# Attention, routed experts and a mixer on one core: shares stored as rows, and work moved around the first gather

## The reference

```python
# 1: attention of 8 heads of 64, plain within |i - j| < 4, plus attention on means of 4 tokens
out_d = sm_attn(q_d, k_d, v_d); out_up = np.repeat(out_d, factor, axis=2)
attn_out = out_up + out_local
# 2: one of 8 experts per token; a token keeps the expert before it where its gate is >= 0.5
e = fresh_e if s == 0 or local_gate[b, s] < 0.5 else prev_e
p = softmax(logits[b, s])
out[b, s] = p[e] * (np.maximum(x[b, s] @ w1[e], 0.0) @ w2[e])
# 3: a mixer over tokens, then over channels
h = np.maximum(xt @ w_tok1, 0.0) @ w_tok2; u = x + h.T
return u + np.maximum(u @ w_ch1, 0.0) @ w_ch2
```

## Time and profile before

| | us |
|---|---|
| median of 3 runs (lowest, highest) | 935.54 (933.09, 939.22) |
| profiled execution | 937.33 |
| its span | 935.6 |
| TensorE busy in the span | 864.2 |
| VectorE, ScalarE, GpSimd busy | 453.7, 349.0, 232.5 |

### The profile page before, as it was taken

One profiled execution on the slowest core, in us unless ns is written; L12 is line 12 of the kernel. 1 busy time (PEld: TensorE's weight loads), 2 busy tenths in 40 slices (PEclk: granted clock), 3 DMA queues, 4 the chain that ended last, 5 costly groups with the idle time before them and its releaser, 6 DMA issues.

```text
span 935.6 us, 13425 instructions
## 1 busy us (share of the span) xinstructions
PE 864.2 (92%) x4498; PEld 720.4 (77%) x4499; DVE 453.7 (48%) x892; ACT 349.0 (37%) x874; POOL 232.5 (25%) x356
## 2 busy tenths in 40 slices
PE   5889889787699979999999978999999999999998
PEld 3666767656478868888887866899989989999997
DVE  6896978878653434255563537412122353122211
ACT  5666776755153433345563433111111121111110
POOL 6886876763322122221221220000000000000000
PEclk9999999999599989999999997999999999999999
DMA  9658785530161945164554614001001020000000
GB/s 158 114 95 198 151 175 113 150 108 11 52 210 63 196 151 186 46 214 159 197 189 138 199 48 147 1 1 67 2 11 58 1 68 1 1 34 1 34 1 34
DMA packets 98703, 88.41 MB, mean 94 GB/s; under 512 B 67808, under 2 KB 73568, under 8 KB 98656
## 3 DMA queue, kind: packets, MB, share of 16 engines
q1 hardware_dynamic: 94816, 75.22, 30.0%
q0 software_dynamic: 3840, 12.59, 4.5%
HBM read 72.31 MB, written 15.48 MB: 94 GB/s over the span
## 4 chain that ended last, share of the span: by engine, by line
PE 71%; DVE 13%; DMA 5%; issue 4%; POOL 3%; ACT 2%; SPq 1%; POOLq 0%; DVEq 0%; ACTq 0%
PE bank L1625 16%; PE bank L1627 16%; PE bank L1626 16%; PE bank L1683 4%; PE bank L1684 4%; PE bank L1690 4%; DVE xT L1129 2%; PE bank L1674 2%; DVE aT L1107 2%; DMA y_dr<-ysb,snow 2%; DVE kB L1072 2%; DVE nm L1085 1%; PE bank L1463 1%; DMA stage<-in_moe_w 1%; PE bank L1633 1%
## 5 line engine op out<-in xcount | busy, mean ns | idle before, releaser
L1356 DVE SCALAR_TENSOR_TENSOR h2l<-bank,h2h 128x384 fp32r<-128x384 f32 x72 | 40.2, 559 | 190.0 <-ACT h2h L1010 190.0
L1010 ACT ACTIVATE h2h<-bank 128x384 fp32r<-128x384 f32 x72 | 35.4, 492 | 229.7 <-PE bank L1627 229.7
L1625 PE MATMUL bank<-uTh,W 128*128 128x384 f32 x288 | 98.1, 340 | 0.0
L1626 PE MATMUL bank<-uTl,W 128*128 128x384 f32 x288 | 97.5, 338 | 0.0
L1627 PE MATMUL bank<-uTh,W 128*128 128x384 f32 x288 | 97.1, 337 | 0.0
L1627 PE MATMUL bank<-W,h2l 128*128 128x512 f32 x216 | 84.5, 391 | 0.0
L1625 PE MATMUL bank<-W,h2h 128*128 128x512 f32 x216 | 84.3, 390 | 0.0
L1626 PE MATMUL bank<-W,h2h 128*128 128x512 f32 x216 | 84.1, 389 | 0.0
L1683 PE MATMUL bank<-W,hTh 128*128 128x512 f32 x184 | 77.4, 420 | 0.0
L1305 DVE TENSOR_TENSOR W<-stage,W 128x1024 fp32r<-128x1024 f32 x56 | 66.6, 1220 | 20.8 <-ACT W L959 20.6
L1311 DVE TENSOR_TENSOR hTl<-bank,hTh 128x512 fp32r<-128x512 f32 x46 | 31.8, 691 | 91.9 <-ACT hTh L968 91.9
(11 more groups left out here) (218 smaller groups left out, 1812.9 us busy)
## 6 DMA issues: line engine op xcount, KB each, us to landing
stage<-in_moe_w SPq DMA_DIRECT2D x56, 512.0 KB, 4.6
vl<-in_v SPq DMA_DIRECT2D x40, 128.0 KB, 3.7
qraw<-in_q SPq DMA_DIRECT2D x32, 144.0 KB, 5.4
kraw<-in_k SPq DMA_DIRECT2D x32, 144.0 KB, 5.0
v<-in_v SPq DMA_DIRECT2D x8, 576.0 KB
ub<-y_dr SPq DMA_DIRECT2D x18, 256.0 KB, 4.7
out<-ob SPq DMA_DIRECT2D x18, 256.0 KB, 2.6
x_dr<-xrow SPq DMA_DIRECT2D x16, 256.0 KB, 3.7
```

What stands on the lines that cost most here:

```text
L1010: act.activation(dst, bank[bk][:, 0:width], ACT.Relu).then_inc(relu_hi, 1)
L1356: dve.scalar_tensor_tensor(dst, bank[bk][:, 0:width], 0.0, hi.bitcast(F32), ALU.max, ALU.subtract).then_inc(bank_free, 1)
L1625: pe.matmul(ps, ah, bh, start=first, stop=False)
L1626: pe.matmul(ps, ah, bl, start=False, stop=False)
```

## The change

1. The last head pair keeps two of its seven halves (in units 1 and 4). ScalarE makes its five later ones (`LATE_SPLITS`) behind the exponentials of the shares, VectorE three behind the first gather's indices and two behind `x_lo(0)`. TensorE starts expert 0 with the first eight halves (w1) and waits for the others before its down products.
2. `best_of(0)` moves from iteration 70 to 73, `choose(0)` and `less_max(0)` behind the loop. In the drain the three pieces of logits stand together, ahead of rows 1 and 2.
3. The code is multiplied in with `hot_lane`, as second operation of the comparison, no longer into `hot_col`. VectorE makes 18 lanes, GpSimd six.
4. `keep_busy(3)` before the marks are turned, `keep_busy(8)` behind the sums.
5. Shares are computed behind the late halves. TensorE turns them before expert 6, ScalarE copies them and stores 24 rows of 96; SyncE reads 18 rows of 128, TensorE turns them, ScalarE copies them to `prob`. Experts 6 and 7 stand behind the loop over pairs. `t2h` is made behind expert 6 on ScalarE. GpSimd's memsets and first extra gather wait for what they need in a new order: the gather for `route_done`, the memsets for `prob_done`.

```diff
@@ side_work
-                work += [("logits", b, 0), ("rows", b, 1), ("logits", b, 1), ("logits", b, 2), ("rows", b, 2)]
+                work += [("logits", b, 0), ("logits", b, 1), ("logits", b, 2), ("rows", b, 1), ("rows", b, 2)]
@@ split_work
-    if hb == NHB - 1 and u < 7:
-        return [9 + u]
+    if hb == NHB - 1 and u in (1, 4):
+        return [9 + (1, 4).index(u)]
...
+LATE_SPLITS = [range(11, 14), range(14, 16)]
...
-DVE_LANES = 17
+DVE_LANES = 18
@@ SyncE
-            sp.wait_ge(prob_done, 1)
-            sp.dma_start(p_dr.rearrange("(k p) -> p k", p=QP), shares[:, :, :].rearrange("p b t -> p (b t)"),
-                         allow_slow_non_contiguous=True).then_inc(p_out, 16)
...
-            sp.dma_start(prob[:, :], p_dr.rearrange("(t p) -> p t", p=P), allow_slow_non_contiguous=True
-                         ).then_inc(p_in, 16)
+            sp.dma_start(probT[:, :], p_dr.rearrange("(t p) -> t p", p=P)).then_inc(p_in, 16)
@@ GpSimd
-                pool.tensor_scalar(hot_lane[:, k, :], lane_row[0:QP, :], lane[:, k:k + 1], None, ALU.is_equal
-                                   ).then_inc(hot_lane_pool, 1)
+                pool.tensor_scalar(hot_lane[:, k, :], lane_row[0:QP, :], lane[:, k:k + 1], id_code[:, k:k + 1],
+                                   ALU.is_equal, ALU.mult).then_inc(hot_lane_pool, 1)
...
-            pool.wait_ge(prob_done, 1)
+            pool.wait_ge(route_done, 1)
             pool.wait_ge(xg_turned, 1)
             gather(1, 0)
+            pool.wait_ge(prob_done, 1)
@@ ScalarE
             act.activation(ex[:, :, :], lm[:, :, :], ACT.Exp).then_inc(ex_done, 1)
+            for cs in LATE_SPLITS:
+                for c in cs:
+                    split_hi(c)
...
+            act.wait_ge(shares_turned, 1)
+            act.activation(sharesT[:, :], bank[7][0:NK, 0:QP], ACT.Copy).then_inc(sharesT_done, 1)
+            act.wait_ge(sharesT_done, 1)
+            act.dma_start(p_dr.rearrange("(k p) -> k p", p=QP), sharesT[:, :]).then_inc(p_out, 16)
+
+            expert(E - 2, (1, E - 1))
             act.activation(t2h[:, :, P // 2:P // 2 + S], raw2[:, :, P // 2:P // 2 + S], ACT.Copy
                            ).then_inc(tok_hi, 1)
-
-            expert(E - 2, (1, E - 1))
...
+            act.wait_ge(prob_turned, 1)
+            act.activation(prob[:, :], bank[7][:, 0:NT], ACT.Copy).then_inc(prob_ready, 1)
@@ VectorE
-                if g == RA + 7:
+                if g == NU + 1:
                     dve.wait_ge(experts_numbered, 1)
                     best_of(0)
-                if g == RA + 8:
-                    choose(0)
-                    less_max(0)
+            choose(0)
+            less_max(0)
...
-            tt(hot_col[:, :, :], hot_col[:, :, :], bc(id_code[:, :].unsqueeze(2), wide), ALU.mult
-               ).then_inc(hot_col_done, 1)
...
             dve.sem_inc(route_done, 1)
+            for c in LATE_SPLITS[0]:
+                split_lo(c)
...
             x_lo(0)
+            for c in LATE_SPLITS[1]:
+                split_lo(c)
+            dve.wait_ge(ex_done, 1)
...
@@ TensorE
                 if g == NU + 5:
+                    pe.wait_ge(route_const, 1)
+                    keep_busy(3, bank[5])
                     turn_marks()
...
             mm.then_inc(summed, 1)
+            keep_busy(8, bank[5])
...
-            pe.wait_ge(raw0_lo, 2 * CPE)
+            pe.wait_ge(raw0_lo, CPE)
...
                     pe.wait_ge(y_copied, j + 1)
+                    pe.wait_ge(raw0_lo, 2 * CPE)
                     down_hi([0, 1])
...
-            with pe.Fori(0, E // 2) as eh:
+            with pe.Fori(0, E // 2 - 1) as eh:
                 expert(2 * eh, 0)
                 expert(2 * eh + 1, 1)
...
+            pe.wait_ge(prob_done, 1)
+            pe.transpose(bank[7][0:NK, 0:QP], shares[:, :, :].rearrange("p b t -> p (b t)"), ident[0:QP, 0:QP]
+                         ).then_inc(shares_turned, 1)
+            expert(E - 2, 0)
+            expert(E - 1, 1)
...
+            pe.wait_ge(p_in, 16)
+            pe.transpose(bank[7][:, 0:NT], probT[:, :], ident[0:NT, 0:NT]).then_inc(prob_turned, 1)
             pe.wait_ge(moe_done, 1)
```

More of the change, by code:

```diff
@@ L139 @@
 KD, KF, KC = DM // P, F // P, CH // P
-SPLIT_AT = {c: w for w, c in enumerate(c for g in range(NU) for c in split_work(g))}
+SPLIT_AT = {c: w for w, c in enumerate([c for g in range(NU) for c in split_work(g)] +
+                                       [c for cs in LATE_SPLITS for c in cs])}
 LAST_TILES = [range(0, 3), range(3, 5), range(5, 6)]
@@ L267, in build @@
         id_high = sb("id_high", M, [QP, KT, B])
-        id_code = sb("id_code", M, [QP, NK], F16)
+        id_code = sb("id_code", M, [QP, NK])
         within = sb("within", M, [QP, E, B])
@@ L273, in build @@
         shares = sb("shares", M, [QP, B, KT])
+        sharesT = sb("sharesT", M, [NK, QP])
+        probT = sb("probT", M, [NT, P])
         gnow = sb("gnow", M, [P, 1], I32)
@@ L407, in build @@
         route_done = sem("route_done")
+        shares_turned, sharesT_done = sem("shares_turned"), sem("sharesT_done")
         p_out, p_in = sem("p_out"), sem("p_in")
+        prob_turned, prob_ready = sem("prob_turned"), sem("prob_ready")
         lm_done, ex_done = sem("lm_done"), sem("ex_done")
@@ L1028, in _ @@
                 hi_mix(m)
+            act.wait_ge(prob_turned, 1)
+            act.activation(prob[:, :], bank[7][:, 0:NT], ACT.Copy).then_inc(prob_ready, 1)
             act.wait_ge(moe_done, 1)
-            act.wait_ge(p_in, 16)
+            act.wait_ge(prob_ready, 1)
             for i in range(NK5):
@@ L1249, in _ @@
             wide = [QP, NK, NSL2]
-            step(tt(hot_col[:, :, :], bc(col_row[0:QP, :].unsqueeze(1), wide), bc(col[:, :].unsqueeze(2), wide),
-                    ALU.is_equal))
-            tt(hot_col[:, :, :], hot_col[:, :, :], bc(id_code[:, :].unsqueeze(2), wide), ALU.mult
-               ).then_inc(hot_col_done, 1)
+            tt(hot_col[:, :, :], bc(col_row[0:QP, :].unsqueeze(1), wide), bc(col[:, :].unsqueeze(2), wide),
+               ALU.is_equal).then_inc(hot_col_done, 1)
             dve.wait_ge(lane_done, 1)
             for k in range(DVE_LANES):
-                dve.tensor_scalar(hot_lane[:, k, :], lane_row[0:QP, :], lane[:, k:k + 1], None, ALU.is_equal
-                                  ).then_inc(hot_lane_dve, 1)
+                dve.tensor_scalar(hot_lane[:, k, :], lane_row[0:QP, :], lane[:, k:k + 1], id_code[:, k:k + 1],
+                                  ALU.is_equal, ALU.mult).then_inc(hot_lane_dve, 1)
             dve.wait_ge(inverted, 1)
@@ L1325, in _ @@
             x_lo(0)
+            for c in LATE_SPLITS[1]:
+                split_lo(c)
+            dve.wait_ge(ex_done, 1)
+            step(dve.tensor_reduce(dn[:, 0, :], ex[:, :, :].rearrange("p t (b e) -> p (t b) e", e=E), AX.X, ALU.add))
+            step(dve.tensor_scalar_add(dn[:, 1, :], dn[:, 0, :], 1e-9))
+            step(dve.reciprocal(dn[:, 2, :], dn[:, 1, :]))
+            step(tt(pex[:, :, :], ex[:, :, :], seq[:, :, :], ALU.mult))
+            step(dve.tensor_reduce(ps_[:, :], pex[:, :, :].rearrange("p t (b e) -> p (t b) e", e=E), AX.X, ALU.add))
+            step(tt(shares[:, :, :].rearrange("p b t -> p t b"), ps_[:, :].rearrange("p (t b) -> p t b", b=B),
+                    dn[:, 2, :].rearrange("p (t b) -> p t b", b=B), ALU.mult))
+            dve.sem_inc(prob_done, 1)
             def expert(e, split):
@@ L1388, in _ @@
             dve.wait_ge(moe_done, 1)
-            dve.wait_ge(p_in, 16)
+            dve.wait_ge(prob_ready, 1)
             for i in range(NK5):
@@ L1560, in weigh, with keep_busy @@
                 mm.then_inc(o_done, 1)
+            def keep_busy(n, bk):
+                for _ in range(n):
+                    pe.matmul(bk[:, :].rearrange("p (r c) -> p r c", r=4), ones_b[:, :],
+                              bc(ident_b[:, :].unsqueeze(1), [P, 4, P]), start=True, stop=True)
             def side_pieces(g):
@@ L1634, in turn_slot @@
                 mm.then_inc(xg_turned, 1)
-            def keep_busy(n):
-                for _ in range(n):
-                    pe.matmul(bank[7][:, :].rearrange("p (r c) -> p r c", r=4), ones_b[:, :],
-                              bc(ident_b[:, :].unsqueeze(1), [P, 4, P]), start=True, stop=True)
-            keep_busy(10)
+            keep_busy(10, bank[7])
             turn_slot(0)
-            keep_busy(6)
+            keep_busy(6, bank[7])
             pe.wait_ge(route_done, 1)
-            pe.wait_ge(raw0_lo, 2 * CPE)
+            pe.wait_ge(raw0_lo, CPE)
             def expert(e, par):
```

11 lines of the change are left out of this document (removed).

## The result

| us | median | lowest to highest | before, same chip | ratio, 95% interval |
|---|---|---|---|---|
| the changed kernel | 927.35 | 925.49 to 929.35 | 934.94 | 0.9906 (0.9879 to 0.9934) |
| once more, another chip | 924.84 | 923.66 to 925.96 | 937.07 | 0.9871 (0.985 to 0.9892) |
| a third time, another chip | 925.13 | 923.47 to 928.76 | 936.55 | 0.9878 (0.9858 to 0.9898) |

The change makes the kernel 0.9 to 1.3% faster: 7.6, 12.2 and 11.4 us in the three comparisons, where 14.2 was forecast. All three medians lie in the forecast's range of 917 to 927.5 us, the first by only 0.15 us; the forecast gain itself was too large in every comparison. Its profiled execution (929.35 us) is the slowest of its five.

The account below looks back on a forecast made before the run. TensorE, busy 864.2 of 935.6 us, was taken as the bound, so only its gaps and low-clock stretches could be won. Terms -4.2 - 1.6 - 0.1 - 0.8 - 7.8 + 0.3 = -14.2 gave 921.3 us, range 917 to 927.5.

Parts of the forecast that it names:

- Attention's end: Last head pair: five of VectorE's seven halves leave and `best_of(0)` moves, -4.2 us to its last copy of weights.
- The clock in the drain: TensorE after attention: without the 2.48 us gap its clock doesn't fall to 1.2 GHz, -1.6 us, bounded by 0.
- Logits before rows and three products: Before the marks are turned: logits 0.5 us earlier, row block and three idle products make TensorE 0.4 late, -0.1 net.
- The codes: Routing: `hot_col` loses its second operation, GpSimd makes six lanes instead of seven, at the mean price, -0.8 us.
- The bound +2.1: Routing's lanes: GpSimd's six all at its slowest price, 1.27 us each, 7.6 us together, costing 2.1 us.
- Late halves and shares: First expert slots: late halves and shares fit into idle time of ScalarE and VectorE, 0 us, far bound +0.7.
- Behind it are its 1.57 us of idle time: VectorE after `x_lo(0)`: 3.5 us more work is covered by idle times of 1.57 and 2.26 us, 3.8 together.
- Shares as rows: Slot at 322.74 us: storing rows instead of single elements removes the scatter's stall, -7.8 us, bounds -8.2 and -5.
- Small additions: Two more transposes on TensorE with waits, +0.3 us; ScalarE's copies and `t2h` lie in time when nothing waits for them.
- The stall stays: Rival: loads of token and expert weights in flight, not the store, held the scatter; +7.8, 929.1 us, chance 0.10.
- The clock falls elsewhere: Rival: TensorE idles before the gather lands, first slot at half speed (2.9 us), 0.9 lost before marks; 925 us, chance 0.12.
- Slower: Rival: the clock falls in the first slot and stays low; at 50 us it costs 25, giving 946 us, chance 0.02.

Follow-up runs that it names:

- e2: The changed kernel with the six operations on shares put back ahead of `x_lo(0)`, behind the first three late halves; 926.14 us, ratio 0.9878.
- e1: The kernel before with only the storage of the shares changed to rows (turned, stored as 24 rows of 96), `t2h` behind expert 6; 932.40 us, ratio 0.9938.
- e7: The changed kernel with the shares stored and read by single elements again, by SyncE ahead of expert 3's loads; 933.04 us, ratio 0.9965.
- e12: The kernel before, run and profiled once more with nothing changed; 937.35 us.

## Why the prediction was right, and where it wasn't

**Attention's end, -4.2: right.** -4.46 in the mean, the same within 0.03 us in all 11 profiles with the edit, between the two bounds.

**The clock in the drain, -1.6: the step failed.** To the first product with `wg` it gave 1.15, since those units run at 2.4 GHz. But "Without the gap I expect no fall" was wrong: the clock fell all the same, 2 to 5 us further on, with TensorE busy, and took the products with `wg` or the idle ones. To the marks 0.30 us went back, net -0.85. A fall was allowed for, here by the bound 0 and in the first slot by a rival of 0.12, but not expected.

**Logits before rows and three products, -0.1: right in the mean only.** The 0.5 from the earlier logits is seen where the clock holds (6.62 to 6.09 us) and lost where it doesn't (6.86, 7.81). The idle products cost up to 0.9 us before the marks, and where they cost nothing they gain 0.4 behind them (7.90 against 8.29 us); over nine and five profiles it is 8.20 against 8.29.

**The codes, -0.8: wrong sign.** The step "I take the mean price, since the loop over 128 elements stays one pass" failed. It is +0.28. GpSimd's median went from 0.70 to 0.90 us an operation, VectorE's lanes from 3.10 / 17 = 0.18 to 4.31 / 18 = 0.24 us. The mean of 0.79 that the prediction took mixes three prices: in the kernel before GpSimd's first two lanes take 1.27 and 0.93 us, beside VectorE's two operations on `hot_col`, the next four 0.70, beside VectorE's lanes, and the last 0.60, alone. So one lane less was worth 0.70 and one `hot_col` operation less some 0.2, against 0.2 us more for each of six. The bound +2.1 was far off: GpSimd's six took 0.97 us in the mean. The rule on blocking of the Trainium skill ("SBUF — State Buffer", who interferes with whom) doesn't set the price beside the lanes: both engines are in them at once, from 244.83 to 249.14, and GpSimd takes 0.87 to 0.91 us there against 0.79 for its last, almost alone. Beside `hot_col`, a VectorE operation with two inputs in SBUF, the trace agrees with it: GpSimd's first takes 1.50 us, 0.71 more than alone, and `hot_col` itself 0.84.

**Late halves and shares, 0: failed, +1.2.** The step was "Behind it are its 1.57 us of idle time". From `xTl` to the first low part it is 2.27 us before and 2.22 in e2, which has two halves between; with the six operations there too it is 5.92. So the idle time covered the halves and nothing of the six. It wasn't free time: it holds the loads of the slot's bounds into registers, with what belongs to them 2.0 us, which aren't counted as busy. They run beside the halves, which wait for nothing, and start only behind the last of the six, each of which waits for the one before (lines at e2). The low parts free the buffers of the ring, the last chunks land later, ScalarE stands before one of them, and with it the `relu` that TensorE waits for 1.08 us: this chain was missing in the prediction, which had the last chunk's wait hidden behind products.

**Shares as rows, -7.8: right for its slot,** which falls from 20.1 to 12.3 us; 5.45 us is what all slots together gained. One step in it was too short, with no cost: the scatter there lands not after the median of 2.8 us but after 6.2 to 6.7; TensorE still doesn't wait for the gather. Given back: 1.2 in the second slot; 1.0 near 470 us, where ScalarE issues the store before its first chunk of expert 7, which the part on small additions had as hidden; 0.8 in the mean of three by the late chunk near 310 us; 0.2 by a slot of 13.05 in one profile, not looked into. Against that 0.8 us came from the slot near 490 us (14.19 and 13.46 before; 13.33, 12.53 and 13.23 changed), not forecast.

**Small additions, +0.3:** from the last slot to the end -0.5, less by 0.8 than forecast; not followed further.

**The rivals.** *The stall stays* is refuted by e1 and e7. Two of its readings were off: of the loads in flight only five of ten landed within 9 us, the others after 10.9 to 15.4, and elsewhere scatters issued beside expert loads land in 3.7 to 4.3 us in five cases, not 2.8. *The clock falls elsewhere* came half true: it fell, not in the first slot (12.6 us in all) but in the drain, with 0.9 lost before the marks as that rival has it, and its 925 us is where two of the three medians lie, by a sum of other terms. *Slower* did not happen.

Together: -14.2 forecast, -10.8 in the profiles. Of the 3.4 us, 1.1 are the codes, 0.8 the clock and the logits up to `lane` (0.9 instead of 1.7), 2.35 the slots and 0.2 the start, less 0.8 at the end and 0.3 in attention. The sum's best end was added wrongly: the terms at their best give 16.1 us and not 18. The range held because what was missed stayed small beside the two terms that came as forecast, the stall and attention's end.

## What to carry to other kernels

An engine's idle time ahead of a loop can hold the loads of the loop's bounds into registers, which no busy share counts. Work that waits for nothing runs beside them; a chain of short operations that wait for each other goes on top in full. Work put ahead of the consumer of a ring of buffers is paid one slot later, on another engine, so follow the buffers and not only the engine. A stall that one long transfer explains could be forecast to the tenth in its own slot, though not in the total; terms around a clock that moves between executions need several profiles of both kernels.

## What the runs showed of the hardware

- TensorE's clock fell to 1.2 GHz with no gap just before it: in the changed kernel TensorE is busy in all of 228 to 231 us, most of it in products of 10 columns, and runs at 0.50 from 231.4; its last gap over 0.15 us, one of 0.98, ended at 222.9. In the 14 profiles the first fall in the drain comes 25 to 32 us after the first maxima and ends 3.4 to 20.5 us later; the changed kernel differs from itself by 3 us in where it starts and by 3.4 us in how long it lasts. What sets the place is not shown.
- VectorE's loads of two bounds into registers ahead of the slots take 2.0 us from first to last, aren't counted as busy, and run beside operations that wait for nothing (e2) but not beside a chain of waits (5.92 instead of 2.22 us to the first low part).
- A comparison with a second multiplication by a number per partition costs more than without: 0.24 against 0.18 us on VectorE, 0.90 against 0.70 on GpSimd beside VectorE's lanes and 0.79 against 0.60 alone, for 96 x 128 in 16 bits. GpSimd's first lane, beside `hot_col` on VectorE, takes 1.50 and 1.27 us.
- A store of 2304 single elements lands after 15.9 to 17.1 us, and an indirect scatter issued beside it and the bulk loads after 12.9 to 14.3, where without that store the longest lands after 5.7 to 7.1 (before, e7, e12 against the 11 others) and the median is 2.8.
